# Early counts, reordered vector work and 128-column gate products at the border between attention and experts

## The reference, cut to what matters

```python
cur = np.einsum('bhd,bhe->bhde', u[None] * kt, vt)
y[:, :, t] = np.einsum('bhd,bhde->bhe', rt, state + cur)
state = w[None, :, :, None] * state + np.einsum('bhd,bhe->bhde', kt, vt)
...
expert_idx = np.argmax(x @ w_gate, axis=1)          # x: 1536 x 384, w_gate: 384 x 8
disp[e, counts[e]] = x[i]; pos[i] = counts[e]; counts[e] += 1     # while counts[e] < capacity (384)
y = np.einsum('ecf,efd->ecd', np.maximum(np.einsum('ecd,edf->ecf', disp, w1), 0.0), w2)
out[i] = gate_w[i] * y[expert_idx[i], pos[i]]
...
h = x @ w_in
return (h - np.tanh(h)) @ w_out
```

## Time and profile before

| | us |
|---|---|
| median of 3 runs | 411.19 |
| lowest and highest of them | 410.8 and 417.55 |
| the profiled execution | 410.51 |
| span of the profiled execution, first to last instruction | 408.8 |
| TensorE busy in the span | 384.9 (94%) |
| VectorE busy in the span | 214.2 (52%) |
| mean granted TensorE clock | 0.98 |

### The profile page before, as it was taken

The page is one execution under the profiler, slowest core; times in us unless marked ns, Lnnn a source line. Parts: engine busy times, 40 slices in busy tenths (PEclk is TensorE's granted clock), DMA queues, the critical chain, the costliest instruction groups (busy, mean ns, idle before and its releaser), DMA issues.

```text
span 408.8 us, 10468 instructions
## 1 busy us (share of the span) xinstructions
PE 384.9 (94%) x3738; PEld 373.1 (91%) x3739; DVE 214.2 (52%) x453; ACT 180.9 (44%) x486; POOL 155.7 (38%) x132
## 2 busy tenths in 40 slices
PE   7999898698999999999999899999999999999991
PEld 7777687598999999999999899999999999999991
DVE  7667978574555655555465356615252434343340
ACT  5553456434564665756656454533022313231220
POOL 3966665435877742715517051541002000110002
PEclk9999999689999999999999999999999999999997
DMA  7989986444849478576684527000000000010001
GB/s 246 271 251 269 249 211 220 141 149 154 264 162 285 150 249 261 189 253 192 224 284 158 182 79 226 6 21 38 0 0 19 38 0 0 0 58 0 0 0 65
DMA packets 41541, 56.85 MB, mean 139 GB/s; under 512 B 3584, under 2 KB 39104, under 8 KB 41504
## 3 DMA queue, kind: packets, MB, share of 16 engines
q1 hardware_dynamic: 35936, 46.23, 36.9%
q10 hardware_dynamic: 3600, 5.31, 4.1%
q0 software_dynamic: 1968, 4.83, 3.1%
HBM read 46.23 MB, written 10.13 MB: 138 GB/s over the span
## 4 chain that ended last, share of the span: by engine, by line
PE 58%; issue 18%; POOL 13%; DVE 4%; DMA 2%; ACT 2%; another core or an unknown queue 1%; POOLq 0%; DVEq 0%; SPq 0%; ACTq 0%
POOL w_lo L460 11%; PE ring L1065 9%; PE ring L1067 9%; PE ring L1066 9%; PE pO L1317 8%; PE pO L1316 8%; PE pY L1189 2%; POOL token_of_rank L521 2%; PE ring L1205 2%; PE pA L1140 2%; PE pD L1094 1%; DVE At L880 1%; PE pY L1174 1%; PE pX L1084 1%
## 5 line engine op out<-in xcount | busy, mean ns | idle before, releaser
L460 POOL TENSOR_TENSOR w_lo<-raw_weights,w_hi 128x768 fp32r<-128x768 f32 x40 | 73.5, 1846 | 84.6 <-ACT w_hi L580 84.3
L1007 DVE SCALAR_TENSOR_TENSOR minus_tanh<-square,ring 128x384 f32<-128x384 f32 x64 | 35.5, 554 | 93.5 <-ACT square L730 79.1
L580 ACT ACTIVATE w_hi<-raw_weights 128x768 fp32r<-128x768 f32 x80 | 67.1, 848 | 28.5 <-DMA raw_weights<-w 28.4
L730 ACT ACTIVATE square<-ring 128x384 f32<-128x384 f32 x64 | 31.4, 491 | 94.7 <-DVE h_hi L1017 53.8
L1065 PE MATMUL ring<-yT_hi,w_hi 128*128 x192 | 65.0, 339 | 1.7 <-DVEq L1002 1.7
L1316 PE MATMUL pO<-w_hi,h_hi 128*128 128x384 f32 x192 | 64.9, 338 | 0.0
L1317 PE MATMUL pO<-w_lo,h_hi 128*128 128x384 f32 x192 | 64.8, 338 | 0.0
L1066 PE MATMUL ring<-yT_lo,w_hi 128*128 x192 | 64.8, 338 | 0.0
L1067 PE MATMUL ring<-yT_hi,w_lo 128*128 x192 | 64.8, 338 | 0.0
L1065 PE MATMUL ring<-xT_hi,w_hi 128*128 128x224 f32 x192 | 52.9, 275 | 1.6 <-issue 1.1
L849 DVE TENSOR_TENSOR w_lo<-raw_weights,w_hi 128x768 fp32r<-128x768 f32 x40 | 42.4, 1073 | 22.3 <-ACT w_hi L580 18.7
(11 more groups left out here) (158 smaller groups left out, 744.1 us busy)
## 6 DMA issues: line engine op xcount, KB each, us to landing
raw_weights<-w SPq DMA_DIRECT2D x80, 384.0 KB
x_by_slot<-x ACTq DMA_DIRECT2D x9, 576.0 KB, 4.4
x_expert<-x_by_slot SPq DMA_DIRECT2D x8, 576.0 KB
kv<-kv_by_token SPq DMA_DIRECT2D x22, 192.0 KB, 4.2
rkT<-rk_by_feature SPq DMA_DIRECT2D x18, 192.0 KB, 5.1
rkT<-rk_by_feature SPq DMA_DIRECT2D x3, 512.0 KB, 4.5
x_expert<-x_by_slot SPq DMA_DIRECT2D x1, 384.0 KB
x_by_slot<-x,sloti POOLq DMA_INDIRECT x12, 4.1
```

The source lines that it names most:

```text
L460: pool.tensor_tensor(lo, unit_raw(2, k), hi.bitcast(F32), ALU.subtract).then_inc(w2_ready, 1)
L580: act.activation(hi, unit_raw(what, k), ACT.Copy).then_inc(w1_hi if what == 1 else w2_hi, 1)
L730: act.activation(sq[:, i % 2, :], ring[i % 4][:, 0:CAP], ACT.Square, scale=THIRD ** 0.5, accum_out=sqsum[:, bass.ds(t * (2 * FC) + i, 1)]) ...
L1007: dve.scalar_tensor_tensor(out=nt[:, i % 2, :], in0=sq[:, i % 2, :], scalar=1.0, in1=ring[i % 4][:, 0:CAP], op0=ALU.subtract, op1=ALU.mult ...
```

## The change

- VectorE: `low(0, 1, 0)`, the second quarter of w1, comes behind `output(STEPS - 1)` and no longer ahead of it.
- TensorE: `positions(3)` and the count product come right behind the three products of tile 8; all three products of tile 9 follow them. Before, the first two of tile 9 stood ahead of them.
- A new semaphore `counts_ready` is signalled by VectorE as soon as the integer counts exist; ScalarE's and TensorE's first branch and SyncE's wait for it in place of `meta_ready`. ScalarE waits for `meta_ready` behind its first branch.
- VectorE makes the counts ahead of the scan for the ranks (`kb_in`) and of `low(0, 3, 0)`. The rest of the metadata (kept, off, off_i, tail, tail_i) moves behind `split_x(0, NARROW)` and its branch.
- TensorE: both `keep_warm` calls at the border go. The two products for the ranks (L1232, L1233) move between the second and the third chunk of tiles 10 and 11.
- The gate products stream 128 columns (the 8 gate columns repeated 16 times) into `pD[:, 0:128]` in place of 8; the copy still takes 8.

```diff
--- before.py
+++ after.py
@@ -237,6 +237,7 @@
         cnt_full = sem("cnt_full")
         slots_ready = sem("slots_ready")
         spot_ready = sem("spot_ready")
+        counts_ready = sem("counts_ready")
         meta_ready = sem("meta_ready")
         m_c = sem("meta_chain")
         kb_in = sem("kb_in")
@@ -415,7 +416,7 @@
             for n in range(DIRECT, STEPS):
                 sp.wait_ge(scat[n], 16)
             sp.wait_ge(ring_full, KD)
-            sp.wait_ge(meta_ready, 1)
+            sp.wait_ge(counts_ready, 1)
             with sp.If(tokens_of(sp, 0) > NARROW):
                 sp.wait_ge(wide_full, KD)
             sp.dma_start(xe[:, :, :], expert_rows(1)).then_inc(xe_in, 16)
@@ -684,11 +685,12 @@
                     act.copy(xTh[:, c, 0:cols], ring[c][:, 0:cols]).then_inc(ring_hi, 1)
 
             split_x(0, NARROW)
-            act.wait_ge(meta_ready, 1)
+            act.wait_ge(counts_ready, 1)
             with act.If(tokens_of(act, 0) > NARROW):
                 for c in range(KD):
                     act.wait_ge(wide_full, c + 1)
                     act.copy(xTh[:, c, NARROW:CAP], ring[c][:, NARROW:CAP]).then_inc(wide_hi, 1)
+            act.wait_ge(meta_ready, 1)
 
             def first(j, s, cols):
                 e = j * 2 + s
@@ -894,12 +896,12 @@
                     low(0, 0, 0)
                 if n == STEPS - 1:
                     route1(2, rlink)
-                    low(0, 1, 0)
                 if n in ROUTE2:
                     route2(ROUTE2[n], rlink)
                 if n in ROUTE1:
                     route1(ROUTE1[n], rlink)
             output(STEPS - 1)
+            low(0, 1, 0)
             route2(2, rlink)
             spots_of(8)
             spots_of(9)
@@ -913,25 +915,14 @@
 
 
             link = chained(dve, m_c)
+            dve.wait_ge(cnt_full, 1)
+            link(dve.tensor_tensor(cnt[:, :], pD[:, 0:E], ebase[:, :], ALU.subtract))
+            link(dve.tensor_copy(cnt_i[:, 0:E], cnt[:, :]))
+            dve.sem_inc(counts_ready, 1)
             link(dve.tensor_tensor_scan(rk[:, 1, :], ones[:, 0:STEPS], allf[:, 2, :], 0.0, ALU.mult, ALU.add))
             link(dve.tensor_tensor(rk[:, 2, :], rk[:, 1, :], allf[:, 2, :], ALU.subtract))
             dve.sem_inc(kb_in, 1)
             low(0, 3, 0)
-
-            dve.wait_ge(cnt_full, 1)
-            link(dve.tensor_tensor(cnt[:, :], pD[:, 0:E], ebase[:, :], ALU.subtract))
-            dve.tensor_copy(cnt_i[:, 0:E], cnt[:, :])
-            link(dve.tensor_scalar(kept[:, :], cnt[:, :], float(CAP), None, ALU.min))
-            link(dve.tensor_tensor_scan(off[:, 1, :], ones[:, 0:E], kept[:, :], 0.0, ALU.mult, ALU.add))
-            link(dve.tensor_tensor(off[:, 0, :], off[:, 1, :], kept[:, :], ALU.subtract))
-            link(dve.tensor_copy(off_i[:, :], off[:, 0, :]))
-            dve.sem_inc(meta_ready, 1)
-
-            for i in range(N // CAP):
-                last = dve.tensor_scalar(tail[:, i:i + 1], off[:, 1, E - 1:E], float(i * CAP), float(N), ALU.add,
-                                         ALU.min)
-            link(last)
-            link(dve.tensor_copy(tail_i[:, :], tail[:, :]))
 
             def split_x(base, cols):
                 for c in range(KD):
@@ -945,6 +936,18 @@
                     dve.wait_ge(wide_hi, c + 1)
                     dve.tensor_tensor(xTl[:, c, NARROW:CAP], ring[c][:, NARROW:CAP], xTh[:, c, NARROW:CAP].bitcast(F32),
                                       ALU.subtract).then_inc(wide_done, 1)
+
+            link(dve.tensor_scalar(kept[:, :], cnt[:, :], float(CAP), None, ALU.min))
+            link(dve.tensor_tensor_scan(off[:, 1, :], ones[:, 0:E], kept[:, :], 0.0, ALU.mult, ALU.add))
+            link(dve.tensor_tensor(off[:, 0, :], off[:, 1, :], kept[:, :], ALU.subtract))
+            link(dve.tensor_copy(off_i[:, :], off[:, 0, :]))
+            dve.sem_inc(meta_ready, 1)
+
+            for i in range(N // CAP):
+                last = dve.tensor_scalar(tail[:, i:i + 1], off[:, 1, E - 1:E], float(i * CAP), float(N), ALU.add,
+                                         ALU.min)
+            link(last)
+            link(dve.tensor_copy(tail_i[:, :], tail[:, :]))
 
             link(dve.tensor_tensor(owner[:, :, :], bc(prio[:, :].unsqueeze(1), [P, STEPS, E]),
                                    bc(allf[:, 0, :].unsqueeze(2), [P, STEPS, E]), ALU.is_equal))
@@ -1091,7 +1094,8 @@
                     pe.wait_ge(lg_done, n)
                 pe.wait_ge(xt_done, n + 1)
                 for i in range(KD):
-                    last = pe.matmul(pD[:, 0:E], xT[:, i, :], wgate[:, i, :], start=(i == 0), stop=(i == KD - 1))
+                    last = pe.matmul(pD[:, 0:P].rearrange("p (a e) -> p a e", e=E), xT[:, i, :],
+                                     bc(wgate[:, i, :].unsqueeze(1), [P, P // E, E]), start=(i == 0), stop=(i == KD - 1))
                 last.then_inc(lg_full, 1)
 
             def own_products(n):
@@ -1215,12 +1219,10 @@
             logits(STEPS - 1)
             for c in range(KD):
                 direct(8, c, near, True, False)
-            direct(9, 0, near, False, False)
-            direct(9, 1, near, False, False)
             positions(3)
             pe.matmul(pD[:, 0:E], ones[:, :], upto[:, STEPS, :], start=True, stop=True).then_inc(cnt_full, 1)
-            direct(9, 2, near, False, False)
-            keep_warm(2, ones[:, :], pX[:, 0:P])
+            for c in range(KD):
+                direct(9, c, near, False, False)
             pe.wait_ge(xe_in, 16)
             for c in range(KD):
                 loaded(c, 0, slice(0, P))
@@ -1228,11 +1230,11 @@
             for c in range(KD):
                 direct(10, c, near, False, False)
                 direct(11, c, near, False, True).then_inc(ring_full, 1)
-            pe.wait_ge(kb_in, 1)
-            pe.matmul(pR[:, 96:96 + STEPS], before[:, :], allf[:, 2, :], start=True, stop=False)
-            pe.matmul(pR[:, 96:96 + STEPS], ones[:, :], rk[:, 2, :], start=False, stop=True).then_inc(kb_full, 1)
-            pe.wait_ge(meta_ready, 1)
-            keep_warm(4, ones[:, :], pO[0][:, 0:P])
+                if c == 1:
+                    pe.wait_ge(kb_in, 1)
+                    pe.matmul(pR[:, 96:96 + STEPS], before[:, :], allf[:, 2, :], start=True, stop=False)
+                    pe.matmul(pR[:, 96:96 + STEPS], ones[:, :], rk[:, 2, :], start=False, stop=True).then_inc(kb_full, 1)
+            pe.wait_ge(counts_ready, 1)
             with pe.If(tokens_of(pe, 0) > NARROW):
                 pe.wait_ge(xe_rest_in, 16)
                 pe.wait_ge(ring_done, KD)
```

## The result

Four executions of the changed kernel took 415.72, 417.18, 417.93 and 415.30 us, median 416.45; four of the kernel before beside them had a median of 412.70. The ratio leaves out executions more than 1.5% above the fastest of their kernel and so can differ from that of the medians. It is 1.0096 [1.0051, 1.0141]: slower by 1%, 3.9 us, less than the 2% that was to be told from no change. The median lies above the predicted 408.5 to 412.6. The profiled execution took 415.72 us, its span is 414.0 us against 408.8, the mean granted clock 0.976 against 0.980. Two repeats with 12 executions each (first experiment) gave 1.0011 and 1.0027.

The account below looks back on a forecast made before the run. TensorE's solid expert stage was taken to bind, its start set at the border by data and control, with h_lo binding the fifth group. Profiled 410.51 - 0.14 - 0.71 = 409.66, plus 0.68 for the median: 410.3 us, range 408.5 to 412.6.

Parts of the forecast that it names:

- The swap, at nothing: VectorE, last output ahead of a weight quarter: gains nothing as long as TensorE's signal is late; cost 0.
- The late signal is gone: Rival, chance 0.10: the last output's signal comes at 74.1, the clock hardly falls, expert 0's rows bind; -3.16, 408.0 us.
- 128 columns cost nothing: TensorE's gate products: the stationary load sets the pace at either width, so widening was taken as 0; upper end 7.2 us.
- the 1.4 of the rival: Rival, wide gate products cost after all, 19 ns a record over 72 records: 1.4 us, 411.7; chance 0.07.
- equal paces: Argument for free wide gate products: 8-column records at 0.112 us each, 128-column products by ones at 0.11.
- They bring clock: Wide gate products at the border start dense streaming 1.42 us sooner, so the clock rises sooner: -0.71 us, bounds 0 and -1.6.
- Positions and counts early: Border before the experts: earlier positions and counts let the expert stage begin at 91.27, 1.67 us sooner than 92.94.
- T: End of VectorE's three splits at the border; forecast at 91.17 us and not 91.50.
- Metadata behind the splits: VectorE, 1.51 us moved behind the splits: fifth group at 97.63, TensorE stands about 1.5 us; -0.14 left without the clock.
- The clock holds through the new stand: The sum's assumption at the first expert's fifth group: TensorE's new wait of about 1.5 us got no clock cost.
- the new stand lowers the clock: Rival, chance 0.17: the wait at the first expert's fifth group drops TensorE's clock, costing 2.0 us; 412.3 us.

Follow-up runs that it names:

- first experiment: The changed kernel's same file timed again twice, 12 executions each, against the kernel before: ratios 1.0011 and 1.0027.
- after_more: Changed kernel plus seven idle VectorE subtractions behind the splits, ahead of the rank chain: 418.22 us, ratio 1.0169 to the kernel before.
- the held scatters: Changed kernel with metadata ahead of the splits, and GpSimd's scatters of tiles 4 to 7 held until the last output is written: 412.69 us, ratio 1.0101.
- after_again: The changed kernel run again, file unchanged: 414.38 us, ratio 1.0011 to the kernel before.
- after_narrow2: Changed kernel with gate products of 8 columns again, second run: 413.20 us, ratio 1.0083 to the kernel before.
- before_again: The kernel before against itself, file unchanged: 410.50 us, ratio 1.0026.
- before_sem: The kernel before with one unused semaphore declared, no instruction added: 410.31 us, ratio 1.0003.
- after_meta: Changed kernel with the rest of the metadata (kept to tail_i) moved ahead of the splits: 411.14 us, ratio 0.9941 to the kernel before.
- meta_woven2: Changed kernel with metadata ahead of the splits and the rank chain's first instructions woven between the splits, second run: 411.28 us, ratio 0.9988.

## Why the prediction was right or wrong, point by point

**The swap, at nothing: right.** The wait ahead of the output is there (2.45 us), and undoing the swap changes nothing (1.0022). That the signal is late was read from one execution, and it is so in six profiles of 18. "The late signal is gone" was thus no outcome of the change but of the execution. y11 to the fifth group takes 24.3 us in the mean of the six and 22.0 in that of the ten others without after_more and the held scatters: 2.3 us, for the 3.16 that the rival gave it.

**128 columns cost nothing: wrong in size.** 0.10 us for six and not 0, 1.2 us in all if every group is on the path, close to the 1.4 of the rival. The "equal paces" were misread: 0.112 us is the six records' time up to the next product. From the first record's start to the sixth's, the narrow group takes 0.73 less 0.25 us and the wide one 0.84 less 0.28, which is 0.096 and 0.112 a record. **They bring clock: right in direction.** The step took one rise at the border, 1.42 us sooner, for -0.71. In the first profile the half clock lasts from 83.60 to 87.01, not gone "before 85", but the rise comes 10.2 us behind y11 where it came 12.7 behind it before. The mean clock of 12 executions is higher by 0.007 to 0.012 with wide products, and the gain is rather 1 to 2 us net.

**Positions and counts early: right.** In the first profile y11 to T took 16.76 us, predicted 18.25, though over the 18 profiles this stretch scatters from 14.5 to 19.9; the first expert product stood at T + 0.05 or 0.06 in all twelve profiles with this part of the change, predicted T + 0.1. TensorE's first load of a count started at 90.5, 3.0 us ahead of T, where the prediction needed 3.04; in after_again 2.8 were enough. What this part is worth was overrated: the 1.44 us between T and the start of the stage, which it takes away, is the high end of what the kernel before has, and in its other two profiles h_lo and not the branch set the fifth group.

**Metadata behind the splits: the mechanism right, a term mis-sized.** h_lo at T + 6.41 to the hundredth, the fifth group at T + 6.46 to the hundredth. But the stand was worked out from TensorE being there "at T + 4.93". It was there at T + 4.06. The 4.83 us between the start of the stage and the fifth group were taken from before as if they were work; 0.82 of them was a stop (between the starts at 94.48 and 95.32 in that trace, put down to issue). The same measure is 0.11 to 0.60 in the four other profiles with that order of VectorE's work and a late branch, so it was another chance of one execution. So the stand was 2.40 and not 1.5 us. The text had named that possibility, "2.1 if the short issue gap ... no longer fills it", and then left it in a rival at 0.17.

**The clock holds through the new stand: wrong, and this is the failed step.** The sum had no term for it: TensorE's stand at the fifth group was counted as waiting only, at no cost in clock. All seven profiles with a stand of 2.38 us or more have a stretch at half clock that begins within 1.3 us of the fifth group, after_more's 2.1 us ahead of it; of the eleven with 0.88 or less none has. Of after_narrow2:

```profile
95.00:97.10 2.10, 0.01 (x1) 0.00 (x0) 0.50 (x3) 1.15 (x3) 2.09 (x2) 1.00 0.79 266
97.40:100.60 3.20, 3.20 (x17) 3.20 (x16) 0.95 (x3) 0.36 (x1) 1.20 (x1) 0.50 0.62 165
```

The rival "the new stand lowers the clock" happened, with a price of 1.7 us for the stretch (2.0 predicted), and of 2.1 us from the fifth group to the end in the mean (313.3 against 311.2 over seven and eleven profiles, which overlap: 311.8 to 314.0 and 309.7 to 314.1). Five of the 18, three of the seven and two of the eleven, have one more stretch of 3.4 us at half clock near 231 to 240 us; without these five the means are 313.0 and 310.8. Metadata ahead of the splits takes both away and brings 2.0 us. That this fall follows this stand is shown by the undoing in two runs; how the cost divides, 1.5 us for the fifth group's place behind T and 1.7 for the clock, is worked out from the traces and not shown by a run.

The working of that rival rests on a misread row. The fall of the clock in the kernel before was taken to follow the stand of 2.29 us at 75.8. It came ahead of it, at 75.38, while TensorE was at work:

```profile
72.00:75.38 3.38, 2.53 (x44) 2.17 (x44) 2.90 (x10) 2.02 (x5) 2.61 (x4) 1.00 0.23 84
75.38:75.80 0.42, 0.42 (x3) 0.32 (x2) 0.07 (x1) 0.00 (x0) 0.42 (x1) 0.50 0.93 347
```

So that trace said nothing about how long a stand the clock bears, and it showed that the clock can fall with no long stand in front. That the rival came true with nearly its price is in part luck.

**The range.** 412.6 was the rival's price on top of a median of three executions. Medians of before alone beside the four sets of versions were 413.99, 410.33, 412.56 and 410.90, and its executions lie between 404.6 and 426. Of the first +3.9 us the change owns 0.8 to 3.0 by all three comparisons, and perhaps nothing by the two longer ones; the rest is the luck of few executions, which no step of the working had a term for. In the repeats the wait and the fall at the fifth group, some 3 us together against before_again and before_sem, are for the most part made up elsewhere. The wide products and the earlier start are what the runs offer for that; the sum isn't shown.

**What stays open.** Why the attention loop takes 72.7 to 81.6 us up to y11 by the execution, what makes the output's signal late in some, and why the clock falls behind one stand and not behind another of the same length. No version beats both kernels beyond doubt; after_meta comes nearest (0.9970 [0.9943, 0.9998]).

## What to carry to other kernels

When a stage is started sooner, ask who has to be ready four steps further on: work deferred "behind the critical part" on a second engine can turn into a stand of the first, and on TensorE a stand can be paid twice, in waiting and in clock. Before a distance is carried over from the old trace, take the stops out of it, since the change may remove them, and profile the old kernel more than once to see which distances hold still. And where one kernel's executions spread by some per cent, time the same file twice before explaining a difference of one per cent.

## What the runs showed of the hardware

- TensorE's granted clock fell to 0.50 at the end of a stand of 2.1 us (idle time as printed) or up to 1.3 us behind it, in work that was dense on both sides, for 3.4 us; so it did in all six profiles with such a stand ahead of the fifth group (1.95 to 2.16 us), and not in the eleven with 0.6 us or less of idle time there. In one of 6.1 us it fell inside the stand. The length alone doesn't decide: one of 2.15 us, some 4 us behind the fifth group in meta_woven2, left the clock at 1.00, and of the stops of 1.7 to 2.1 us that all 18 profiles have between 224 and 241 us five were followed by 3.4 us at half clock.
- Columns streamed count for the clock: the same six gate products with 128 instead of 8 columns raised the mean granted clock of the kernel before from 0.973 to 0.983, for 0.10 us a group.
- Two VectorE instructions on 12 columns lasted 1.38 and 1.46 us in place of 0.17 while GpSimd ran a two-input operation.
- From VectorE's integer ranks to the first h_lo VectorE is idle for 1.59 to 1.60 us in fifteen of 18 profiles (register loads and branches stand there), and for 1.85, 1.86 and 2.08 in the others; no reordering shortened it.
